# Where eight long-lived SBUF tiles lie: the three small ones allocated after the five large ones

## The reference

```python
for t in range(S):
    cur = einsum('bhd,bhe->bhde', u * k[t], v[t])
    y[t] = einsum('bhd,bhde->bhe', r[t], state + cur)
    state = w[t][..., None] * state + einsum('bhd,bhe->bhde', k[t], v[t])
```

## Time and profile before

| | |
|---|---|
| median of 3 runs | 1041.33 us (1040.7 to 1042.37) |
| the profiled execution, its own time | 1042.37 us |
| its span, from first to last instruction | 1040.6 us |
| PE busy | 997.7 us, 96% |
| DVE, ACT, POOL busy | 623.3, 246.2, 489.2 us |
| granted TensorE clock, mean | 0.985 |

### The profile page before, as it was taken

How to read it: one execution, slowest core, us unless ns; L and a number is a source line. 1 busy time by engine, 2 the same in 40 slices (tenths; PEclk the granted TensorE clock), 3 DMA queues, 4 the chain that set the end, 5 groups by cost and what they waited for, 6 DMA issues and landing times.

```text
span 1040.6 us, 16737 instructions
## 1 busy us (share of the span) xinstructions
PE 997.7 (96%) x5680; PEld 882.3 (85%) x5680; DVE 623.3 (60%) x1047; ACT 246.2 (24%) x488; POOL 489.2 (47%) x540
## 2 busy tenths in 40 slices
PE   4778988899999999999999999999999999999998
PEld 4778988888888888888888888888888888888988
DVE  7878798988776877778776867444332212121221
ACT  2132312222123121222122212333322212121211
POOL 7656586857574757566674757212010201011111
PEclk9689999999999999999999999999999999999999
DMA  6533312212112120303021220201301010101000
GB/s 200 161 89 96 97 46 77 74 50 96 58 60 63 55 97 3 108 12 133 18 88 34 91 63 5 92 31 61 122 0 61 1 61 8 53 15 45 23 8 31
DMA packets 36221, 64.65 MB, mean 62 GB/s; under 512 B 4928, under 2 KB 22720, under 8 KB 36160
## 3 DMA queue, kind: packets, MB, share of 16 engines
q1 hardware_dynamic: 30288, 52.12, 15.2%
q10 hardware_dynamic: 5872, 11.80, 3.5%
HBM read 54.46 MB, written 9.44 MB: 61 GB/s over the span
## 4 chain that ended last, share of the span: by engine, by line
PE 84%; DVE 5%; POOL 5%; issue 3%; ACT 1%; DMA 0%; SPq 0%; ACTq 0%; POOLq 0%; DVEq 0%
PE ps_sc L503 10%; PE ps_acc L484 8%; PE ps_acc L486 8%; PE ps_acc L485 8%; PE ps_gate L484 6%; PE ps_gate L486 6%; PE ps_val L484 6%; PE ps_gate L485 6%; PE ps_val L486 5%; PE ps_val L485 5%; PE ps_desk L527 3%; PE ps_sc L486 2%; PE ps_sc L484 2%; PE ps_sc L485 2%; POOL kT L1168 2%
## 5 line engine op out<-in xcount | busy, mean ns | idle before, releaser
L503 PEld LDWEIGHTS ps_sc<-rB,kT 128*128 128x128 f32 x1152 | 155.8, 202 | 36.8 <-DVE rB L913 18.0
L503 PE MATMUL ps_sc<-rB,kT 128*128 128x128 f32 x1152 | 162.2, 288 | 25.8 <-DVE A L938 10.6
L1168 POOL TENSOR_TENSOR kT<-kT,wT 128x256 f32<-128x256 f32 x164 | 140.0, 853 | 83.9 <-PE ps_sc L503 56.4
L1236 POOL TENSOR_TENSOR h_lo<-h2f,h_hi 128x512 fp32r<-128x512 f32 x36 | 46.3, 1285 | 247.5 <-ACT h_hi L857 247.5
L1139 POOL TENSOR_TENSOR h_lo<-act_h,h_hi 128x512 fp32r<-128x512 f32 (+1 forms) x83 | 97.7, 1178 | 108.8 <-ACT h_hi L707 104.2
L1175 POOL TENSOR_TENSOR rB<-rB,wT 64x256 f32<-64x256 f32 x144 | 121.1, 841 | 11.3
L913 DVE TENSOR_TENSOR rB<-rB,wT 64x256 f32<-64x256 f32 x144 | 96.1, 672 | 30.4 <-PE ps_sc L503 23.7
L484 PE MATMUL ps_gate<-x_hi,wg_hi 128*128 128x512 f32 (+1 forms) x252 | 97.0, 385 | 8.9 <-DVE act_h L888 6.9
L707 ACT ACTIVATE h_hi<-act_h 128x512 fp32r<-128x512 f32 (+1 forms) x84 | 47.9, 571 | 230.4 <-DVE act_h L891 230.2
L938 DVE COPY_PREDICATED A<-mask,ps_sc 128x512 f32<-128x512 uint8 x120 | 98.9, 824 | 0.0
L484 PE MATMUL ps_acc<-h_hi,wo_hi 128*128 128x512 f32 (+1 forms) x252 | 95.7, 380 | 0.5 <-POOL h_lo L1139 0.3
(11 more groups left out here) (136 smaller groups left out, 2028.7 us busy)
## 6 DMA issues: line engine op xcount, KB each, us to landing
kT<-in_k_channels SPq DMA_DIRECT2D x24, 256.0 KB, 3.4
wT<-in_w_channels SPq DMA_DIRECT2D x24, 256.0 KB, 4.0
rB<-in_r_channels SPq DMA_DIRECT2D x48, 128.0 KB, 2.6
kL<-in_k_tokens SPq DMA_DIRECT2D x24, 192.0 KB, 2.4
rL<-in_r_tokens SPq DMA_DIRECT2D x24, 192.0 KB, 2.5
vL<-in_v_tokens SPq DMA_DIRECT2D x24, 192.0 KB, 2.4
x_scratch<-x1s SPq DMA_DIRECT2D x6, 768.0 KB, 4.4
xn<-x_scratch SPq DMA_DIRECT2D x6, 768.0 KB, 4.3
```

The source lines that it names most:

```text
L503: last = mm(ps_sc[:, j, q * T:(q + 1) * T], kT[2 * duo + j][:, q, :], rights, start=True, stop=True)
L1168: tt(half(kT[b][:, :, :], h, 0), half(kT[b][:, :, :], h, 0), block_decay(b, h, 1), ALU.mult).then_inc(k_scaled, 1)
```

## The change

The three small tiles gcol, ident and warm are allocated after the five large ones instead of ahead of them. No instruction, loop, wait or DMA is added or taken away.

```diff
-        gcol = sb("gcol", [P, KC])
-        ident = sb("ident", [P, P])
-        warm = sb("warm", [P, 1])
         x_hi = sb("x_hi", [P, KC, TOK], F32R)
         x_lo = sb("x_lo", [P, KC, TOK], F32R)
         xn = sb("xn", [P, B, DM])
         xf = xn[:, :, :].rearrange("p b n -> p (b n)").rearrange("p (c t) -> p c t", t=TOK)
         x1s = sb("x1s", [P, KC, TOK])
         act_h = sb("act_h", [P, 2, TOK])
+        gcol = sb("gcol", [P, KC])
+        ident = sb("ident", [P, P])
+        warm = sb("warm", [P, 1])
 
         phase1 = ExitStack()
```

## The result

The changed kernel takes 1050.77 us (median of 4 runs, 1048.66 to 1051.33), against 1041.01 us of the kernel before beside it (4 runs, 1039.99 to 1042.37): ratio 1.0097, interval 1.0084 to 1.0111. It is slower by 0.97%, outside the predicted range. The profiled execution took 1051.68 us with a span of 1049.9 us, 9.3 longer than before, at a granted clock of 0.984 (0.985 before).

The account below looks back on a forecast made before the run. PE was taken to bound the kernel, busy 997.7 of 1040.6 us; all terms (TensorE's reads, other engines, DMAs, small tiles) were 0, so the forecast stayed 1041.3 us, range 1039.1 to 1043.5.

Parts of the forecast that it names:

- The 42.9 us of PE's idle time: Whole kernel: all that PE ever stands idle, so nothing off PE can give back more than that.
- Rival C's head: First 200 us: shifted engine collisions give 1040.4 to 1042.2; nearly all within 0.88, bad and good ends within 0.06 each.
- the prediction's list of those for moved tiles: PE's waits for work on moved tiles: L888 6.9 us, L1028 1.5 us and L1040 0.9 us only.
- 0.04 us by the prediction's estimate: DMA rows of 6144 bytes: 198 beats from residue 192, 196 from 128; 1% of a 4.3 us landing, hidden.
- TensorE's reads: 2484 matmuls reading moved tiles: cost change taken as 0, bounds 1 ns each, 2.5 us either way.
- rival A: TensorE's reads of x_hi and x_lo get dearer at the new residue: 1043.8 at 1 ns; 0.06 with another rival's bad end.
- L527 as a witness: L527's vL slices run through residues 192, 128, 64, 0 modulo 256; median 275 ns taken as showing no residue dearer.
- Its list of signs: Signs in the profile after; last, some SBUF unit may tell addresses apart at 128 or 256 bytes for long streams.
- with the 800 us after the head stretched evenly: Sign of dearer x reads: x_hi and x_lo groups 1 ns or more longer, h's not, evenly after the first 200 us.

Follow-up runs that it names:

- 1 to 5: Changed kernel with 64 bytes before weights 1.0092, before all tiles 1.0083, only x_hi/x_lo moved 1.0100, only others moved 1.0001; kernel before with all 64 up 0.9988.
- 11: Changed kernel with 192 bytes of padding behind warm, x_hi kept at its new place: 1041.60 us, ratio 1.0006.
- 13: Standalone matmul trains, operand and weights shifted together, or weights alone: 226.8 ns a step together; weights alone 32 up 233.3, 192 up 228.9.
- 9: Standalone kernel, sixteen trains of 180 matmuls of 512 columns, moving operand's start shifted in 16-byte steps against the weights: 226.7 to 234.6 ns a step.
- experiment 7: Kernel before with gaps (256, 64, 64) ahead of w1, w2, w3, giving phase 2 distances 0, 192, 128: 1045.97 us, ratio 1.0043.

## Why the prediction was wrong

**What held.** The 42.9 us of PE's idle time stayed (43.8). DVE, ACT and POOL have their durations, and no new row stands among PE's waits. Rival C's head took no visible part: of the 3.2 us by which phase 2 starts later, the steps and the idle time place 4.0 + 0.3 - 1.4 - 0.7 + 0.9 = 3.1. One wait was left out of the prediction's list of those for moved tiles, 1.0 us for x_hi at L741; it is 1.0 us in both kernels. The loads of xn still land after 4.3 us. For the change of the residue from 192 to 128 the Trainium skill's rule (DMA: Bandwidth & Descriptors, section on how a descriptor splits into AXI transactions) would have given 0.04 us by the prediction's estimate. The rule speaks of what a DMA reads, and the loads of phase 2 only write xn; it bears on the stores, which read x1s (192 before, 128 after) and land after 4.4 us before and 4.3 after. With 0.1 us of resolution the rows neither bear it out nor speak against it.

**The step that failed** is the one headed "TensorE's reads": "I take 0. The bounds are the difference of the two means, 1 ns". What came is rival A's: the matmuls that read x_hi and x_lo got dearer, and h's did not. The prediction even had the pair in half a clause ("two streams (moving operand and weights) meet"), but laid the cost on the new residue of x itself, which the runs rule out. Its size was bounded by rows that could not show it, in two places.

First, the rows compared were all of one kind. x_hi against wg and h_hi against wo lie 28672 and 36864 bytes apart, both 0 modulo 256. The prediction noted that all operands start at the same residue, and concluded from this "that the distance is free". But equal residues make the distance modulo 256 zero everywhere, so the rows said nothing on the distance either: of the two readings the chip follows the one that was thought to be settled. The move of 576 bytes changed it from 0 to 192 for every matmul that reads x.

Second, L527 as a witness. Its vL slices do run through four distances, since they step by 192 bytes while A's slices are 512 apart. But L527 has 48 columns, and within its groups it steps by 111 to 112 ns, just as L503 does with 128 columns; its mean duration is 284 ns before and after. So the length of their reading is not what sets their step, and they cannot tell what a read costs. The prediction called this "the weakness of this row" and gave it the weight all the same.

**The size.** The term taken as 0, with 2.5 us as its end, measured 8.9 us from the starts: 6.2 in phase 2, where the step of an undisturbed train goes from 226.7 to 233.3 ns (972 x 6.67 = 6.5 at most), 4.0 for 512 columns in the passes, 1.4 back for 256 columns. That the end for rival A was 1 ns where 6.7 was possible is what put the result outside the range. Its list of signs ended on the right one, a grain of 128 or 256 bytes that the trace could not exclude, and gave it no price. The rival's picture "with the 800 us after the head stretched evenly" was off as well: phase 2 is stretched by 2.2% (6.1 of 282.4 us) and all that comes before by 3.2 us, since the passes keep their h matmuls and the ladder's, gain on 256 columns, and have shorter groups, which each start on irregular steps.

**Shown and only argued.** That the distance modulo 256 between moving operand and weights decides is shown, by 1 to 5, 11 and 13; the curve for 512 columns by 9 and 13. The loads themselves take 187 to 188 ns in the median at every distance. That it is the load of the next weights meeting the running matmul's reads is only argued: it is the one moment at which both tiles are read. A train that keeps its weights, which would have tested it, was not run. Why the curve has its shape (240 as good as 0, 16 not, 64 in between) is open. All of it is measured for fp32r operands alone.

The Trainium skill (TensorE: Matmul & The Clock Gate, section "Step-by-step: what each phase is for") says: "Loading the next tile's weights doesn't steal SBUF read bandwidth from the running matmul." At s = 0 the trace has 226.7 ns a step, and no run here splits that into causes; at other distances the step is up to 234.6 ns with nothing else changed, which that sentence has no place for. The measurement decides: a step is up to 7.9 ns longer depending on where the two tiles lie. Whether the load takes that time from the running matmul, no run here shows.

## What to carry to other kernels

Where long trains of fp32r matmuls bound a kernel, work out (start of the moving tile - start of its weights) modulo 256 for every pair, and repeat it when any tile allocated between them changes its size: here 0 is the best for 512 columns (240 equals it), 6.7 ns a matmul better than 192 or 128, though at 256 columns 192 is 6.5 ns better than 0, and 192 bytes of padding made the changed order whole. When two rows are compared to show that a property doesn't matter, check that they differ in it, and that the instruction's duration depends on it at all. Read the cost of a pipelined matmul from its starts and not from its duration.

## What the runs showed of the hardware

- The step of a 512-column fp32r matmul, with new weights for every matmul, depends on the distance of its two operands in SBUF modulo 256 bytes: 226.7 ns at 0 and at 240, 228.9 at 64, 231 to 234.6 at the other multiples of 16.
- At 256 columns it goes the other way: 120.0 ns at 0, 113.5 at 192. At 384 columns 173.4 at 0 and 176.7 at 96.
- Many mean steps come close to multiples of 6.67 ns: 113.5, 120.0, 173.4, 226.7 and 233.3 are 17, 18, 26, 34 and 35 of them. Others, such as 228.9 and 231.1, lie between two. 6.67 ns is 16 clocks at 2.4 GHz, the upper level, at which these stretches run.
- A group at distance 0 that follows on others at another distance took seven irregular steps (224 to 236 ns) before it was back at 226 to 227, in experiment 7. In the passes of the kernel before, where groups of nine alternate with the ladder's short matmuls, the steps within a group stay irregular to its end, mostly 224 to 236 ns after the first.
